# The low part of w_out made on GpSimd in tile 0, and the second convolution ended one block earlier

## The reference, cut to what matters

```python
# x: 4 x 4096 x 192, weight_gen: 4 x 4096 x 8 heads x 7 taps
w = softmax(weight_gen)                          # over the 7 taps
out = einsum('bshk,bskhg->bshg', w, x_unf)       # a convolution over 7 tokens, its taps made per token and head
x = out.reshape(16384, 192)
xn = x / sqrt(mean(x * x) + 1e-6) * rms_g
g, val = xn @ w_gate, xn @ w_val                 # 192 -> 1536 each
result = (g * sigmoid(g) * val) @ w_out          # 1536 -> 192
```

## Time and profile before

| | |
|---|---|
| Time, median of 3 runs | 1299.43 us (1298.48 to 1301.11) |
| The profiled execution: its own time | 1299.58 us |
| its span, first to last instruction | 1297.4 us |
| busy: PE, DVE, ACT, POOL | 98%, 77%, 51%, 3% |
| granted TensorE clock, mean | 1.000 |
| tile 0's blocks | about 24 to 65 us of the span |

### The profile page before, as it was taken

The page is one execution under the profiler, slowest core; times in us unless marked ns, Lnnn a source line. Parts: engine busy times, 40 slices in busy tenths (PEclk is TensorE's granted clock), DMA queues, the critical chain, the costliest instruction groups (busy, mean ns, idle before and its releaser), DMA issues.

```text
span 1297.4 us, 32473 instructions
## 1 busy us (share of the span) xinstructions
PE 1273.1 (98%) x13544; PEld 1240.3 (96%) x13544; DVE 1001.0 (77%) x1511; ACT 663.9 (51%) x1428; POOL 42.8 (3%) x76
## 2 busy tenths in 40 slices
PE   8989899999999999999999999999999999999998
PEld 6978899999999999999999999999999999999998
DVE  6888887877887777887877877777877777877643
ACT  5445455564455654455564455544455544455543
POOL 1000000000000000000000000000000000000000
PEclk9999999999999999999999999999999999999999
DMA  9001222212212112112112122122122121121010
GB/s 299 29 16 54 68 68 69 67 45 68 55 39 68 52 60 58 49 56 68 52 60 56 38 69 68 44 68 56 38 68 69 44 68 56 38 68 38 14 38 14
DMA packets 19644, 76.31 MB, mean 59 GB/s; under 512 B 3119, under 2 KB 4783, under 8 KB 19374
## 3 DMA queue, kind: packets, MB, share of 16 engines
q1 hardware_dynamic: 18798, 73.08, 18.9%
q10 hardware_dynamic: 704, 1.18, 0.4%
HBM read 38.07 MB, written 12.58 MB: 39 GB/s over the span
## 4 chain that ended last, share of the span: by engine, by line
PE 86%; DVE 6%; ACT 3%; issue 3%; DMA 1%; ACTq 0%; POOL 0%; DVEq 0%
PE up_ps L766 55%; PE out_ps L806 21%; PE out_ps L810 9%; DVE h L649 2%; DVE y L225 1%; DMA raw<-in_moe_w_val 1%; DVE prod L223 1%; DVE h_lo L675 1%; ACT silu L458 1%; PE up_ps L715 1%; ACT L458 0%; ACT xn L400 0%; ACT L439 0%; ACT xn L392 0%; PE up_ps L720 0%
## 5 line engine op out<-in xcount | busy, mean ns | idle before, releaser
L766 PE MATMUL up_ps<-xT,w_hi 64*128 64x512 f32 x4608 | 816.2, 392 | 8.5 <-DVE h L649 5.4
L766 PEld LDWEIGHTS up_ps<-xT,w_hi 64*128 64x128 f32 x4608 | 527.2, 184 | 25.9 <-issue 8.6
L766 PE MATMUL up_ps<-xT,w_lo 64*128 64x512 f32 x2304 | 502.5, 387 | 0.0
L806 PE MATMUL out_ps<-wo,h_hi 64*128 64x384 f32 x3072 | 465.0, 356 | 7.1 <-issue 2.4
L810 PE MATMUL out_ps<-wo,h_lo 64*128 64x192 f32 x3072 | 437.2, 247 | 0.0
L649 DVE TENSOR_TENSOR h<-up_ps,silu 128x512 f32<-128x512 f32 x384 | 264.6, 689 | 209.0 <-ACT silu L458 205.9
L467 ACT ACTIVATE h_hi<-h 128x512 fp32r<-128x512 f32 x384 | 242.5, 631 | 346.4 <-DVE h L649 333.6
L806 PEld LDWEIGHTS out_ps<-wo,h_hi 64*128 64x128 f32 x3072 | 357.5, 184 | 11.2 <-issue 3.3
L810 PEld LDWEIGHTS out_ps<-wo,h_lo 64*128 64x128 f32 x3072 | 362.4, 187 | 0.9
L458 ACT ACTIVATE silu<-up_ps 128x512 f32<-128x512 f32 x384 | 227.9, 594 | 246.0 <-PE up_ps L766 237.5
L675 DVE TENSOR_TENSOR h_lo<-h,h_hi 128x512 fp32r<-128x512 f32 x384 | 263.7, 687 | 36.1 <-ACT h_hi L467 35.9
(11 more groups left out here) (77 smaller groups left out, 302.1 us busy)
## 6 DMA issues: line engine op xcount, KB each, us to landing
x_buf<-in_x SPq DMA_DIRECT2D x30, 960.0 KB, 4.7
xT<-xT SPq DMA_DIRECT2D x90, 256.0 KB, 3.9
result<-last SPq DMA_DIRECT2D x32, 384.0 KB, 2.3
taps<-in_weight_gen SPq DMA_DIRECT2D x1, 3136.0 KB, 18.4
raw<-in_moe_w_gate SPq DMA_DIRECT2D x3, 384.0 KB, 9.3
raw<-in_moe_w_val ACTq DMA_DIRECT2D x3, 384.0 KB, 12.2
last<-in_moe_w_out SPq DMA_DIRECT2D x1, 1152.0 KB, 18.1
x_first<-in_x SPq DMA_DIRECT2D x2, 384.0 KB, 10.8
```

The costliest lines, as they stand in the source:

```text
L766: mm = nc.tensor.matmul(ps[:, banks, :], w[rows, s, cols], xT[rows, t, s, part, :], start=(at == 0), stop=ends)
L806: nc.tensor.matmul(out_ps[:, j, 0:2 * D], h_hi[rows, g % HB, cols], wo[rows, g, :, :].rearrange("p a d -> p (a d)"), start=(g == 0 and k < ...
```

## The change

`wo_low` leaves DVE's list and goes to GpSimd's, both halves of it, between the first and the second `inverse_rms`. The operation, its operands and its semaphores are the same: GpSimd waits for `wo_high(n)` and then subtracts. Of the second convolution's 13 steps on DVE, block 1 now has one (none before), block 7 two (one before) and block 9 none (two before); the other blocks have what they had.

```diff
+            def wo_low(n):
+
+                pool.wait_ge(w_hi_done, SLOTS + 1 + n)
+                fs = slice(n * FB // 2, (n + 1) * FB // 2)
+                nc.gpsimd.tensor_tensor(wo[:, fs, 1, :], raw_out[:, fs, :], wo[:, fs, 0, :].bitcast(F32),
+                                        ALU.subtract).then_inc(wo_lo_done, 1)
+
             inverse_rms(0)
+            wo_low(0)
+            wo_low(1)
             for T in range(1, 5):
                 inverse_rms(T)
...
-            def wo_low(n):
-                fs = slice(n * FB // 2, (n + 1) * FB // 2)
-                dve.wait_ge(w_hi_done, SLOTS + 1 + n)
-                nc.vector.tensor_tensor(wo[:, fs, 1, :], raw_out[:, fs, :], wo[:, fs, 0, :].bitcast(F32),
-                                        ALU.subtract).then_inc(wo_lo_done, 1)
...
-            seconds = [0, 0, 1, 1, 2, 2, 2, 1, 2, 2, 0, 0]
+            seconds = [0, 1, 1, 1, 2, 2, 2, 2, 2, 0, 0, 0]
...
                         if f == 0:
                             w_low(1, 0)
-                        if f == 1:
-                            wo_low(0)
                         if f in (2, 3):
                             w_low(1, f - 1)
-                        if f == 7:
-                            wo_low(1)
                         second_conv(sum(seconds[:f]), sum(seconds[:f + 1]))
```

## The result

The changed kernel takes 1303.69 us in the median of 7 runs (1301.99 to 1304.32), the kernel before 1299.08 in 7 runs beside it (1298.48 to 1301.11). The ratio is 1.0025 with an interval of 1.0015 to 1.0036, so 1.9 to 4.7 us slower; the medians are 4.6 apart and the fastest runs 3.5, which is how far times alone can be trusted here. Forecast were +3.3 us and 1302.7. The profiled execution has a span of 1300.4 and a time of 1302.37.

A forecast was written before the change was run, and what follows sets the result against it. PE was taken to set tile 0's pace with DVE barely ahead; two GpSimd holds less the end's gain, 2.5 + 1.55 - 0.6 = +3.45 (other order +2.8), taken as +3.3, gave 1302.7 us, range 1298.3 to 1305.0.

The forecast's parts named there:

- What bounds: Tile 0: PE sets the pace, DVE is half a microsecond ahead, so a 2 us delay of DVE cannot stay hidden.
- The lead of 0.66: Tile 0, project 4 and 5: `h_lo` of block 5 ends at 45.81, 0.66 us before PE needs it at 46.47.
- GpSimd's duration, 2.5 us: Each half of `wo_low`, 1152 elements at 2.16 ns, was estimated to take GpSimd 2.5 us.
- The direction that no row showed: Tile 0: GpSimd reading SBUF holds DVE operations with two SBUF inputs for as long as it streams, 2.5 us.
- Who gets through first: Near 30.1 us GpSimd and `h_lo` of block 0 both want to read; GpSimd first gives +3.45, `h_lo` first +2.8.
- the middle term: Second half, convolution step at 39.95: DVE loses 2.5, of which 0.95 were ahead, so PE stands still for 1.55 us.
- The other order: `h_lo` of block 0 reads before GpSimd, which starts under `h` of block 1: 1.2 + 2.2 - 0.6 = +2.8 us.
- The end of the tile, -0.6: Tile 0's end: `h` of blocks 10 and 11 starts earlier, so the squares and all that follows come 0.6 us earlier.
- The line that was drawn at 0.2%: About 0.2% (2.6 us, 1302.0) is what a measurement of this kernel can tell from no change.
- A: Rival for tile 0: GpSimd takes nothing from DVE, so -0.6 us or 1298.8, not slower; chance 0.28.
- C: Rival for tile 0: GpSimd always yields to DVE's two-input SBUF reads and ends late; +6 us, 1305.4; chance 0.06.
- D: Rival for tile 0: the clock falls in a PE stop of 2.5 us; no size given; chance 0.03.

The follow-up runs named there:

- second half only: Changed kernel with only the second half of `wo_low` on GpSimd, the first back on VectorE; `h` of block 0 to tile 1's first square 34.91 us, before 33.50.
- the copy: Changed kernel with each GpSimd subtraction replaced by a copy of w_out's high part; `h` of block 0 to tile 1's first square 33.90 us, before 33.50.
- start under `h`: Changed kernel with GpSimd also waiting for `h_lo` of blocks 0 and 4; `h` of block 0 to tile 1's first square 36.48 us, before 33.50.
- write-only kernel: Changed kernel with GpSimd zeroing a spare tile and the low part in place of each subtraction; 1299.19 us, ratio 0.9997 against the kernel before.

## Why the prediction was right

- **What bounds.** PE sets the pace of tile 0 and VectorE is about half a microsecond ahead, none at hidden 3. Confirmed: PE waited for `h` ahead of hidden 3. The lead of 0.66 ahead of project 4 and 5 was rather 0.5: with the second half only, 0.51 of the hold stayed hidden.
- **GpSimd's duration, 2.5 us,** from the slopes of a zeroing and a select. Measured: 2.68 for the instruction when nothing is in its way, 2.37 to 2.51 of hold. The size is right, the way to it was in part luck. It took each input read to cost the same 0.67 ns per element, so the copy, which reads one, should have lasted 1.49 x 1152 = 1.7 us. It lasted about 1.18 (the estimate above), 0.1 more than the zeroing's 1.07, and the second input then adds 1.5. One step was too large, the other too small, and they came near the right sum.
- **The direction that no row showed,** that GpSimd's reading holds DVE as DVE's holds GpSimd's. It was taken without a row of this kernel for it, and it carries the forecast. Shown by the changed trace, and narrowed by experiments, each with the instructions tried: operations of DVE with two inputs in SBUF are held, those with one in PSUM are not; a subtraction and a copy on GpSimd's side hold, a zeroing doesn't; the hold is per instruction.
- **Who gets through first.** I left open whether `h_lo` of block 0 or GpSimd goes first and took +3.3 between the two sums. GpSimd went first: 2.5 + 1.55 - 0.6 = 3.45 was the right sum, and 2.47 + 1.58 - 0.59 = 3.46 was measured. That the middle term fits to 0.03 is luck: the hold was 2.37 and not 2.5, and the lead that hid part of it was 2.37 - 1.58 = 0.79 and not 0.95. The other order was made by hand (start under `h`, for both halves) and cost +2.98 where the sum said +2.8, but not by the same terms: 1.69 at the first half where the sum had 1.2, and 1.89 at the second where it had 2.2.
- **The end of the tile, -0.6.** Measured -0.59, and -0.58 alone.
- **The time.** The distance grew by 3.46 where +3.3 was taken. The median of the runs is 1303.69 where 1302.7 was forecast, but runs of one kernel spread over more than 2 us, so that neither confirms nor refutes a term. The line that was drawn at 0.2% lies inside the measured interval (0.15% to 0.36%): that the kernel is slower is shown, that it is slower by more than 0.2% only the trace says.
- **Rivals.** A (nothing held) is what the write-only kernel does, and what the subtraction doesn't. C (GpSimd yields always) falls: DVE's rows are stretched, GpSimd's are only 3.09 and 3.25. D (the clock falls in the stop): the windows at PE's stop, 31 to 33 us, and all behind it up to 60 show a granted clock of 1.00. The granted clock of the 7 timed runs lies at 0.997 to 0.999 in the mean; how much of the spread between them is due to the stop was not tried.

## What to carry to other kernels

GpSimd is no free second elementwise engine beside VectorE: a subtraction that cost VectorE 1.27 us held it for 2.4 on GpSimd. By these runs work is moved there at no cost only if it reads nothing from SBUF, or if VectorE meanwhile works with one input in PSUM, or has a lead as long as GpSimd's instruction. Look for the price in the durations of the other engine's instructions, not in its idle times, and ask first how far ahead the engine is that you relieve.

## What the runs showed that I had not expected

- A GpSimd copy of 1152 elements holds VectorE for 0.83 to 0.94, a subtraction of the same size for 2.37 to 2.51 where VectorE was ready as soon as GpSimd began to read: the second input costs more than the first. A zeroing of 1152 elements on 128 partitions takes 1.07, and holds nothing.
- Between two GpSimd instructions already queued a waiting VectorE instruction gets in, and the other way round.
- The granted clock was at 0.57 from 24 to 28 us in two of the eleven profiles and at 1.00 there in the others. In the one of them without a stop of PE behind it, block 4 came half a microsecond late.
